# Multiplying by the values one group earlier in banded attention, and splitting the first projection weights on other engines and at other times

## The chip, the cores and the metric

The kernel runs as one program on one core of a Trainium2 chip. The metric is the device time of one execution in microseconds. The engines are PE (matrix products, with PEld for its weight loads), DVE (vector), ACT (scalar), POOL (GpSimd) and SP, which here only issues DMAs. Each engine takes its own instructions in order and meets the others through semaphores.

## The reference

Three layers follow one another. The first is what the change touches most: attention with a band of 96 keys and 8 global keys. The second mixes four attention experts, the third is an MLP.

```python
scores = scale * q @ k^T;  scores += -slope_h * distance
a = softmax(where(is_global | is_local, scores, -1e9))
x = a @ v                                  # B=2, H=8, S=768, D=64
for e in range(4):                         # second layer, D=512, Hd=64
    q, k, v = x @ wq[e], x @ wk[e], x @ wv[e]
    ye = softmax(causal(scale * q @ k^T)) @ v @ wo[e]
    out += gate_e * ye                     # top 2 of 4
u = out + mixed(out);  result = u + relu(u @ w_ch1) @ w_ch2
```

## The kernel before

**The work of the first layer.** Two heads make a pair and eight pairs are worked through. The 768 queries of a pair are six tiles of 128, each called a unit, so there are 48 units (`N_UNIT`); two units make a duo, and there are 24 duos (`N_DUO`). The band of a unit is 256 keys wide, except for the first unit of a pair, which has 128. So of every three duos the first is a little smaller.

**The stages of a duo.** PE computes scores (`scores`, line 1228). DVE adds the bias and takes the row minimum of the negated scores (`attend`, line 844). ACT takes the exponential and the sum (line 609). DVE inverts the sum (`safe` and `inverse`, lines 869 and 875) and POOL multiplies by the inverse (`divide`, line 545). PE transposes (`transposes`, line 1241) into `ps_t`. Each unit is then copied from `ps_t` to `probT`: this is `evac`, line 618 on ACT for every fourth unit and line 862 on DVE for the other three. So a duo of even number has one evacuation on each of the two engines, and a duo of odd number has both on DVE. PE multiplies by the values (`values`, line 1261) into `ps_o`, and ACT and DVE write the result to `xh` (line 630) and `xl` (line 882), its rounded part and the rest, since all later products take a sum of three products of such halves (`split_product`, line 1209).

**The order around the change.** It is written out by hand as one loop over `d` on each engine, and each engine runs through its own iterations `d`. Iteration `d` of PE holds `scores` of duo `d`, `values` of duo `d-4` and `transposes` of duo `d-2`, in that order. Iteration `d` of DVE holds the evacuations of duo `d-3`, the four `attend` of duo `d`, the inverse for duo `d-1`, and `x_lo` of duo `d-5`. Iteration `d` of ACT holds its evacuation for duo `d-3`, `x_hi` of duo `d-5` and the exponentials of duo `d`.

**The end of the layer.** From iteration 24 on PE interleaves the first projections of the second layer: keys from `wk` and then queries from `wq`, each for queries 0 to 511 (`LO`) and 512 to 767 (`HI`), by `project_first`. Then come eight transposes of `wo` (line 1484) and the value projections.

**The weights.** A weight comes by DMA to `wraw` or `nat`, and is split in a rounded and a remaining part: `split` on POOL, a cast (line 503) and a subtraction (line 495). The first halves of `wk` and `wq` are four such splits, put between POOL's divisions by `SPLIT_AT`. `wl_done` counts finished splits, so the constants `WK_0`, `WQ_0`, `WV` and so on name how many must be done. SP loads keys and values of pair `p` in turn and puts the weights between them.

Of the kernel before, what the change touches and what calls it, by code (L numbers as in the profile page):

```python
# [21 lines left out]
P = 128  # L22
# [110 lines left out]
def build(nc, t, out):  # L133
    ctx = ExitStack()
    with ctx:
# [145 lines left out]

        def by_unit(x):

            return x.rearrange("p k (f n) -> p k f n", f=2)
# [25 lines left out]
        woT_done, woT_hi, woT_lo = sem("woT_done"), sem("woT_hi"), sem("woT_lo")  # L310
        w1_in = [sem("w1_in0"), sem("w1_in1")]
# [30 lines left out]
        def _(sp):  # L342
# [43 lines left out]
            def load_first_weights():  # L386

                load_qk("wk", qk_first, 0, 0, wk_in)
                load_qk("wq", qk_first, P, 0, wq_in)
                load_wv()  # L390

            def load_late_weights():

# [13 lines left out]
            sp.dma_start(ident[:, :], t["ident"]).then_inc(ident_in, 16)  # L407
            load_values(0)
            load_keys(1)
            load_values(1)  # L410
            with sp.If(is_narrow(sp)):
                for p in range(2, B * HP):
                    load_keys(p)
                    load_values(p)
                    if p == 3:
                        load_first_weights()
                    elif p == 5:
                        load_constants()
                load_late_weights()
            with sp.Else():  # L420
                load_first_weights()
# [33 lines left out]
            def load_w1(j):  # L455

                if j == 0:
                    sp.wait_ge(wl_done, WQ_0)
# [34 lines left out]
        def _(pool):  # L493
# [3 lines left out]
            rqk = wraw[:, 0, 0:KT * 256].rearrange("p (k n) -> p k n", k=KT)  # L497
# [9 lines left out]
            def split_weight(n):  # L507

                if n < WQ_0:

                    of_q = n // 2
                    pool.wait_ge(wq_in if of_q else wk_in, 16)
                    k = slice(2 * (n % 2), 2 * (n % 2) + 2)
                    split(n, rqk[:, k, of_q * P:(of_q + 1) * P], qk_h[:, k, 1 - of_q, 0:P], qk_l[:, k, 1 - of_q, 0:P])
                elif n < WV:
                    k = n - WQ_0
# [32 lines left out]
            pool.wait_ge(one_done, 1)  # L549
            with pool.If(is_narrow(pool)):  # L550
                for d in range(N_DUO + 1):
                    if 1 <= d <= N_DUO:
                        divide(d - 1)
                    if d in SPLIT_AT:
                        split_weight(SPLIT_AT[d])
                pool.wait_ge(norm_done, 2 * N_UNIT)
            with pool.Else():
                for n in range(WQ_0):
                    split_weight(n)
            for n in range(WQ_0, WQK_1):  # L560
# [44 lines left out]
        def _(act):  # L605
# [1059 lines left out]
```

## Time and profile before

| | us |
|---|---|
| median of the runs | 455.48 |
| lowest and highest of three | 455.08, 455.73 |
| the profiled execution, own time | 455.48 |
| its span | 453.7 |
| PE busy | 441.6 (97%) |
| DVE, ACT, POOL busy | 188.5, 166.4, 174.8 |
| chain that ended last, on PE | 95% |

The profiled execution took as long as the median. Its span leaves out 1.8 us around the work. The duos of the first layer run up to about 76 us from the span's start, the interleaved projections to 91, the experts to about 210 and the MLP to the end. Busy time of PE is modelled from pipelined records, so 100% busy in a stretch does not by itself say that PE could go no faster; the start times of its groups say more.

### The profile page before, as it was taken

Reading aid. Unit: us, or ns where it says so; the run is one execution under the profiler, and the core shown is the slowest. Engines: PE = TensorE matmul, PEld = TensorE weight load, DVE = VectorE, ACT = ScalarE, POOL = GpSimd, SP = SyncE. Lnnn points to the kernel's source line nnn. Section 1 sums busy time; section 2 is a strip of 40 time slices with the busy share of each in tenths; the row PEclk is TensorE's granted clock in tenths of the full one; section 3 lists DMA queues with packets and bytes.
Section 4 is the critical chain, followed back from the end, with each engine's and each line's share of the span. In section 5 each row is a group of like instructions: output and inputs, shape, how many; then the busy total and the mean of one; then the engine's idle time right before and its main releaser. Section 6 shows DMA issues by size and latency. Waiting matters only on the chain.

```text
span 453.7 us, 8487 instructions
## 1 busy us (share of the span) xinstructions
PE 441.6 (97%) x3194; PEld 367.8 (81%) x3194; DVE 188.5 (42%) x615; ACT 166.4 (37%) x451; POOL 174.8 (39%) x247
## 2 busy tenths in 40 slices
PE   4999999999999999999999999999999999999996
PEld 3677777887787887667998888888888888888885
DVE  5799998265533634553351222221222122222112
ACT  4898886142643644756331011111012101111102
POOL 0777788806951555775011212222211121122210
PEclk9999999999999999999999999999999999999999
DMA  8797981100020011110101011110111022311003
GB/s 264 231 278 241 265 247 48 49 2 0 4 93 0 1 48 48 46 48 1 48 23 48 25 46 46 48 44 29 46 46 48 2 92 92 94 47 48 25 0 139
DMA packets 29949, 33.47 MB, mean 74 GB/s; under 512 B 9204, under 2 KB 19444, under 8 KB 29908
## 3 DMA queue, kind: packets, MB, share of 16 engines
q1 hardware_dynamic: 29474, 32.40, 23.9%
q8 instruction: 26, 0.43, 0.4%
q10 hardware_dynamic: 434, 0.52, 0.3%
q14 instruction: 15, 0.12, 0.1%
HBM read 29.77 MB, written 3.15 MB: 73 GB/s over the span
## 4 chain that ended last, share of the span: by engine, by line
PE 95%; ACT 1%; DMA 1%; issue 1%; DVE 1%; SPq 0%; POOL 0%; ACTq 0%
PE ps_s L1209 27%; PE ps_o L1209 25%; PE ps_t L1209 12%; PE ps_t L1241 5%; PE ps_s L1228 5%; PE ps_o L1261 5%; PE ps_s L1440 5%; PE ps_o L1473 4%; PE ps_t L1456 4%; PE ps_o L1385 1%; DMA kT<-in_k 1%; DVE prob L844 0%; ACT probT L681 0%; PE ps_o L1374 0%; ACT prob L609 0%
## 5 line engine op out<-in xcount | busy, mean ns | idle before, releaser
L495 POOL TENSOR_TENSOR fl<-fraw,fh 128x512 fp32r<-128x512 f32 x32 | 41.3, 1292 | 177.9 <-DVE fh L1151 177.9
L793 ACT ACTIVATE hidh<-ps_o 128x768 fp32r<-128x768 f32 x32 | 26.0, 813 | 175.8 <-PE ps_o L1209 175.8
L609 ACT ACTIVATE prob<-prob,smin 128x256 f32<-128x256 f32 (+3 forms) x144 | 77.6, 541 | 33.5 <-DVE smin L844 32.8
L1192 DVE SCALAR_TENSOR_TENSOR hidl<-ps_o,hidh 128x768 fp32r<-128x768 f32 x32 | 30.6, 957 | 93.0 <-ACT hidh L793 93.0
L545 POOL TENSOR_SCALAR prob<-prob,sinv,one 128x256 f32<-128x256 f32 (+1 forms) x96 | 50.5, 540 | 24.3 <-DVE sinv L875 24.1
L572 POOL TENSOR_SCALAR prob<-prob,sinv,gate 128x128 f32<-128x128 f32 (+5 forms) x48 | 34.0, 717 | 53.0 <-DVE sinv L895 52.9
L1209 PE MATMUL ps_s<-hidh,fl 128*128 128x512 f32 x128 | 50.4, 394 | 0.0
L1209 PE MATMUL ps_s<-hidl,fh 128*128 128x512 f32 x128 | 50.2, 392 | 0.0
L1209 PE MATMUL ps_s<-hidh,fh 128*128 128x512 f32 x128 | 49.7, 388 | 0.0
L1151 DVE CAST fh<-fraw 128x512 fp32r<-128x512 f32 x32 | 14.4, 449 | 66.5 <-PE ps_t L1209 66.4
L1209 PE MATMUL ps_o<-xh,w_late 128*128 128x512 f32 (+1 forms) x160 | 41.6, 334 | 0.0
L844 DVE CUSTOM_DVE_ANT_0 prob<-ps_s,bias 128x256 f32<-128x256 f32 (+1 forms) x96 | 34.4, 397 | 6.2 <-PE ps_s L1228 5.9
L844 DVE CUSTOM_DVE_ANT_0 prob<-ps_s,causal 128x128 f32<-128x128 f32 (+5 forms) x48 | 29.2, 614 | 18.7 <-PE ps_s L1440 11.9
L1209 PE MATMUL ps_t<-hidh,fh 128*128 128x256 f32 x128 | 35.3, 276 | 0.0
L1209 PE MATMUL ps_t<-hidl,fh 128*128 128x256 f32 x128 | 35.3, 276 | 0.0
L1209 PE MATMUL ps_t<-hidh,fl 128*128 128x256 f32 x128 | 35.3, 276 | 0.0
L681 ACT ACTIVATE probT<-ps_t 128x512 f32<-128x512 f32 (+1 forms) x48 | 24.2, 539 | 21.1 <-PE ps_t L1456 21.1
L1228 PE MATMUL ps_s<-kT,qT 64*128 64x256 f32 (+1 forms) x192 | 28.5, 423 | 2.9 <-DMA kT<-in_k 2.9
L1209 PEld LDWEIGHTS ps_o<-xh,w_late 128*128 128x128 f32 x160 | 28.6, 188 | 3.2
L1209 PEld LDWEIGHTS ps_t<-hidl,fh 128*128 128x128 f32 x128 | 24.0, 188 | 5.4
L1209 PEld LDWEIGHTS ps_t<-hidh,fh 128*128 128x128 f32 x128 | 24.0, 188 | 5.2
L1209 PEld LDWEIGHTS ps_s<-hidh,fl 128*128 128x128 f32 x128 | 24.1, 188 | 4.8
(180 smaller groups left out, 976.8 us busy)
## 6 DMA issues: line engine op xcount, KB each, us to landing
fraw<-in_w SPq DMA_DIRECT2D x32, 256.0 KB, 2.6
wraw<-in_w SPq DMA_DIRECT2D x8, 512.0 KB, 3.3
kT<-in_k SPq DMA_DIRECT2D x16, 224.0 KB, 3.8
vN<-in_v SPq DMA_DIRECT2D x8, 384.0 KB, 4.1
out<-prob SPq DMA_DIRECT2D x12, 256.0 KB, 2.7
qT<-in_q SPq DMA_DIRECT2D x7, 384.0 KB, 3.3
vB<-in_v SPq DMA_DIRECT2D x8, 192.0 KB, 4.2
kT<-in_k SPq DMA_DIRECT2D x7, 128.0 KB, 3.4
```

Source lines behind the costliest of these rows:

```text
L495: return pool.tensor_tensor(lo, raw, hi.bitcast(F32), ALU.subtract)
L545: pool.tensor_scalar(x, x, sinv[:, s:s + 1], one[:, 0:1], ALU.mult, ALU.mult).then_inc(norm_done, 1)
L572: pool.tensor_scalar(x, x, sinv[:, col + par:col + par + 1], gate[:, NT * b + i, e:e + 1], ALU.mult, ALU.mult).then_inc(mnorm_done, 1)
L609: act.activation(prob_s, prob_s, ACT.Exp, bias=smin[:, col:col + 1], scale=-1.0, accum_out=ssum[:, col:col + 1]).then_inc(done, 1)
L681: act.activation(flat[:, n0 * P:n1 * P], ps_t[:, g % 2, 0:(n1 - n0) * P], ACT.Copy).then_inc(mevac_done, 1)
L793: act.activation(hidh[:, f % 2, :], ps_o[:, 0:S], ACT.Relu).then_inc(hidh_done, 1)
L844: dve.tensor_tensor_reduce(out=dst, in0=src, in1=mask, scale=-SCALE, scalar=3e38, op0=ALU.add, op1=ALU.min, accum_out=smin[:, col:col + 1] ...
L1192: dve.scalar_tensor_tensor(hidl[:, f % 2, :], ps_o[:, 0:S], 0.0, hidh[:, f % 2, :].bitcast(F32), ALU.max, ALU.subtract).then_inc(hidl_done, 1)
L1209: last = pe.matmul(dst, a, m, start=start and k == 0, stop=stop and k == n - 1, **kw)
L1228: pe.matmul(a_score[s % 8][:, 0:keys.stop - keys.start], qT[half, p % 2, i * P:(i + 1) * P], kT[half, p % 2, keys], start=True, stop=True, ...
L1241: last = pe.transpose(ps_t[:, u % 2, (n * par + j) * P:(n * par + j + 1) * P], a_prob[s % 12][:, j * P:(j + 1) * P], ident[:, :])
L1261: last = pe.matmul(ps_o[half, at:at + P], v, a_probT[u % 4][:, par, n * P:(n + 1) * P], start=n == 0, stop=own, skip_group_check=True)
```

## The change

Four things change together.

1. `values` of a duo moves one iteration earlier on PE, to `d-3`; `x_hi` and `x_lo` follow, to `d-4`, and the loops on PE, DVE and ACT are one iteration shorter. The evacuations stay where they were, in iteration `d` for duo `d-3`.
2. The two projections `(0, HI)` and `(1, LO)` now stand side by side in iteration 25.
3. The two splits of `wk` are made by POOL before its first division, and the DMA of `wk` is issued before the values of pair 0. The split of `wq` leaves POOL: ACT makes the rounded part in one instruction and DVE the rest in one, both in iteration 24.
4. The constants are loaded after pair 3 and all late weights after pair 4; the cast `mix_hi` on DVE comes one iteration later.

```diff
-WO_BEHIND = {0: (12, 13), 1: (14, 15), VMIX_BEHIND: (16,)}
-WK_0, WQ_0, WV, WQK_1, WO, VMIX = 2, 4, 8, 12, 16, 17
-SPLIT_AT = {13: 0, 16: 1, 19: 2, 22: 3}
+WO_BEHIND = {0: (10, 11), 1: (12, 13), VMIX_BEHIND: (14,)}
+WK_0, WV, WQK_1, WO, VMIX = 2, 6, 10, 14, 15
...
             load_keys(0)
             sp.dma_start(ident[:, :], t["ident"]).then_inc(ident_in, 16)
+            load_qk("wk", qk_first, 0, 0, wk_in)
             load_values(0)
...
                     if p == 3:
-                        load_first_weights()
-                    elif p == 5:
                         load_constants()
-                load_late_weights()
+                    elif p == 4:
+                        load_late_weights()
...
                 if j == 0:
-                    sp.wait_ge(wl_done, WQ_0)
+                    sp.wait_ge(wl_done, WK_0)
+                    sp.wait_ge(wq_lo, 1)
...
             pool.wait_ge(one_done, 1)
+            for n in range(WK_0):
+                split_weight(n)
             with pool.If(is_narrow(pool)):
                 for d in range(N_DUO + 1):
                     if 1 <= d <= N_DUO:
                         divide(d - 1)
-                    if d in SPLIT_AT:
-                        split_weight(SPLIT_AT[d])
...
+            def split_wq_hi():
+                act.wait_ge(wq_in, 16)
+                act.activation(wqk_h[:, :, 0:P], wq_raw, ACT.Copy).then_inc(wq_hi, 1)
...
-                for d in range(N_DUO + 5):
+                for d in range(N_DUO + 4):
                     if 3 <= d < N_DUO + 3 and by_act(2 * (d - 3)):
                         evac(2 * (d - 3))
-                    if d >= 5:
-                        x_hi(d - 5)
+                    if d >= 4:
+                        x_hi(d - 4)
+                    if d == N_DUO:
+                        split_wq_hi()
...
+            def split_wq_lo():
+                dve.wait_ge(wq_hi, 1)
+                dve.tensor_tensor(wqk_l[:, :, 0:P], wq_raw, wqk_h[:, :, 0:P].bitcast(F32), ALU.subtract).then_inc(wq_lo, 1)
...
-                    if d >= 5:
-                        x_lo(d - 5)
+                    if d >= 4:
+                        x_lo(d - 4)
                     if d == N_DUO:
+                        split_wq_lo()
+                    elif d == N_DUO + 1:
                         mix_hi()
...
-                    pe.wait_ge(wl_done, WQ_0 if of_q else WK_0)
+                    pe.wait_ge(*((wq_lo, 1) if of_q else (wl_done, WK_0)))
...
-            first = {N_DUO: [(0, LO)], N_DUO + 1: [(0, HI)], N_DUO + 2: [(1, LO)], N_DUO + 3: [(1, HI)]}
+            first = {N_DUO: [(0, LO)], N_DUO + 1: [(0, HI), (1, LO)], N_DUO + 2: [(1, HI)]}
...
-                for d in range(N_DUO + 4):
+                for d in range(N_DUO + 3):
...
-                    if d >= 4:
-                        values(d - 4)
+                    if d >= 3:
+                        values(d - 3)
```

The order on PE from iteration 3 on, before: `ps_s<-kT,qT` are scores, `ps_t<-ident,prob` transposes and `ps_o<-probT` the product with the values.

```order
L1228 MATMUL ps_s<-kT,qT 128x128 x2
L1228 MATMUL ps_s<-kT,qT 128x256 x2
L1241 MATMUL ps_t<-ident,prob 128x128 x8
L1228 MATMUL ps_s<-kT,qT 128x256 x4
L1261 MATMUL ps_o<-probT,vN 64x128 x6
L1241 MATMUL ps_t<-ident,prob 128x128 x8
```

And the same place with the change, where line numbers are 11 higher:

```order
L1239 MATMUL ps_s<-kT,qT 128x128 x2
L1239 MATMUL ps_s<-kT,qT 128x256 x2
L1272 MATMUL ps_o<-probT,vN 64x128 x6
L1252 MATMUL ps_t<-ident,prob 128x128 x8
L1239 MATMUL ps_s<-kT,qT 128x256 x4
L1272 MATMUL ps_o<-probT,vB 64x128 x2
```

The values of duo 0 moved ahead of the transposes of duo 1, and so for each later duo: between the transposes of a duo and its product with the values there is now one group of scores, where before a whole iteration of three groups lay between them as well.

On DVE, iterations 24 to the end of the loop, before:

```order
L869 TENSOR_SCALAR seps<-ssum 128x4
L875 RECIPROCAL sinv<-seps 128x4
L882 TENSOR_TENSOR xl<-ps_o,xh 128x256
L900 CAST vmix<-vraw 96x768
L862 COPY probT<-ps_t 128x512
L882 TENSOR_TENSOR xl<-ps_o,xh 128x256
L862 COPY probT<-ps_t 128x512 x2
L882 TENSOR_TENSOR xl<-ps_o,xh 128x256 x3
```

and with the change:

```order
L872 TENSOR_SCALAR seps<-ssum 128x4
L878 RECIPROCAL sinv<-seps 128x4
L885 TENSOR_TENSOR xl<-ps_o,xh 128x256
L908 TENSOR_TENSOR wqk_l<-wraw,wqk_h 128x4x128
L865 COPY probT<-ps_t 128x512
L885 TENSOR_TENSOR xl<-ps_o,xh 128x256
L903 CAST vmix<-vraw 96x768
L865 COPY probT<-ps_t 128x512 x2
L885 TENSOR_TENSOR xl<-ps_o,xh 128x256 x2
```

The remaining part of `wq` came in ahead of an evacuation, the cast of `vmix` moved behind it, and one `xl` of the tail moved into the loop.

On POOL, from its memsets to the first divisions, with the change:

```order
L544 MEMSET one 128x1
L500 CAST wqk_h<-wraw 128x2x128
L492 ISA
L492 TENSOR_TENSOR wqk_l<-wraw,wqk_h 128x2x128
L500 CAST wqk_h<-wraw 128x2x128
L492 TENSOR_TENSOR wqk_l<-wraw,wqk_h 128x2x128
L337 TENSOR_LOAD narrow
L337 ISA x2
L548 COMPARE_AND_BRANCH
L541 ISA
L541 TENSOR_SCALAR prob<-prob,sinv,one 128x128 x2
```

Before, the load of `narrow` and the branch followed the memset at once; now two casts and two subtractions, which wait for the DMA of `wk`, stand ahead of them and of the first division.

## Rows read from the trace of the kernel before

**Rows 1.** Busy time by stretch: start:end, length, PE, PEld, DVE, ACT, POOL, PEclk, DMA, GB/s.

```profile
40.76:75.51 34.75, 34.75 (x361) 26.53 (x362) 32.48 (x151) 29.51 (x115) 29.08 (x56) 1.00 0.73 205
```

**Rows 2.** Timeline of PE, products with the values: start, duration, instructions.

```profile
47.55 0.44 PE L1261 MATMUL ps_o<-probT,vB 128*64 128x128 f32 x4
...
50.23 0.44 PE L1261 MATMUL ps_o<-probT,vB 128*64 128x128 f32 x4
...
53.34 0.88 PE L1261 MATMUL ps_o<-probT,vN 128*64 128x128 f32 x12
...
56.24 0.44 PE L1261 MATMUL ps_o<-probT,vB 128*64 128x128 f32 x4
...
58.92 0.44 PE L1261 MATMUL ps_o<-probT,vB 128*64 128x128 f32 x4
...
62.03 0.88 PE L1261 MATMUL ps_o<-probT,vN 128*64 128x128 f32 x12
```

**Rows 3.** Timeline of DVE: evacuations, and first attends, with idle time before them.

```profile
46.61 1.28 DVE L862 COPY probT<-ps_t 128x512 f32<-128x512 f32 x2
...
49.65 0.68 DVE L862 COPY probT<-ps_t 128x512 f32<-128x512 f32 x1
...
51.95 1.29 DVE L862 COPY probT<-ps_t 128x512 f32<-128x512 f32 x2
53.44 0.42 DVE L844 CUSTOM_DVE_ANT_0 prob<-ps_s,bias 128x256 f32<-128x256 f32 x1 [0.21 <-PE ps_s L1228]
...
58.19 1.01 DVE L862 COPY probT<-ps_t 128x256 f32<-128x256 f32 x2
...
61.08 0.69 DVE L862 COPY probT<-ps_t 128x512 f32<-128x512 f32 x1 [0.28 <-PE ps_t L1241]
```

**Rows 4.** Timeline of ACT: its evacuations in the same stretch.

```profile
50.24 0.36 ACT L618 ACTIVATE probT<-ps_t 128x256 f32<-128x256 f32 x1
...
55.89 0.57 ACT L618 ACTIVATE probT<-ps_t 128x512 f32<-128x512 f32 x1
```

**Rows 5.** Timelines of PE in two iterations: the transposes of a full duo.

```profile
19.26 1.23 PE L1241 MATMUL ps_t<-ident,prob 128*128 128x128 f32 x8
...
25.19 1.09 PE L1241 MATMUL ps_t<-ident,prob 128*128 128x128 f32 x8
```

**Rows 6.** The chain that ended last: start, duration, what; the two `HI` projections.

```profile
80.33 1.42 PE ps_s L1209 x12
...
87.35 1.61 PE ps_s L1209 x12
```

**Rows 7.** The start: SP's issue of ident, and ident's time to landing.

```profile
3.56 0.51 SPq L407 DMA_DIRECT2D ident<-in_ident  x1
...
DMA to landing us min/median/max: 4.5/4.5/4.5
```

**Rows 8.** The start: SP's last issue of keys of pair 1, and its time to landing.

```profile
7.66 0.47 SPq L360 DMA_DIRECT2D kT<-in_k  x1
...
DMA to landing us min/median/max: 5.4/5.5/5.6
```

**Rows 9.** Busy time by stretch, columns as in rows 1, at the start.

```profile
8.00:12.00 4.00, 3.71 (x16) 2.47 (x16) 2.12 (x13) 3.14 (x14) 0.23 (x1) 1.00 1.08 333
```

**Rows 10.** The start: timelines of DVE, POOL and PE, with idle time before.

```profile
4.74 0.42 DVE L907 TENSOR_SCALAR near<-rel,cnt 128x384 f32<-128x384 f32 x1 [1.07 <-DMA kpos<-in_kpos]
...
11.77 4.11 POOL L545 TENSOR_SCALAR prob<-prob,sinv,one 128x128 f32<-128x128 f32 x8 [10.79 <-DVE sinv L875]
...
14.39 1.65 PE L1228 MATMUL ps_s<-kT,qT 64*128 64x128 f32 x8
```

**Rows 11.** Timeline of POOL: one weight split, a cast and a subtraction.

```profile
74.44 0.40 POOL L503 CAST wqk_h<-wraw 128x256 fp32r<-128x256 f32 x1
74.92 0.74 POOL L495 TENSOR_TENSOR wqk_l<-wraw,wqk_h 128x256 fp32r<-128x256 f32 x1
```

**Rows 12.** Timeline of DVE in iteration 25: the evacuation, with idle time before it.

```profile
80.36 0.69 DVE L862 COPY probT<-ps_t 128x512 f32<-128x512 f32 x1 [2.62 <-PE ps_t L1241]
```

More of the change, by code:

```diff
@@ L280, in mixed_part @@
             return lambda x: x[:, :, HI], ps_fill.rearrange("p (c n) -> p c n", c=EP)
+        wq_raw = wraw[:, 0, 0:KT * 256].rearrange("p (k n) -> p k n", k=KT)[:, :, P:2 * P]
         def by_unit(x):
@@ L310, in build @@
         woT_done, woT_hi, woT_lo = sem("woT_done"), sem("woT_hi"), sem("woT_lo")
+        wq_hi, wq_lo = sem("wq_hi"), sem("wq_lo")
         w1_in = [sem("w1_in0"), sem("w1_in1")]
@@ L384, in load_wv, with load_late_weights @@
                 sp.dma_start(dst[:, :, 256:260], t["w_gate"]).then_inc(wv_in, 16)
-            def load_first_weights():
-                load_qk("wk", qk_first, 0, 0, wk_in)
+            def load_late_weights():
                 load_qk("wq", qk_first, P, 0, wq_in)
                 load_wv()
-            def load_late_weights():
                 load_qk("wk", qk_raw, 0, 1, wqk_in)
@@ L495, in lo_of @@
                 return pool.tensor_tensor(lo, raw, hi.bitcast(F32), ALU.subtract)
-            rqk = wraw[:, 0, 0:KT * 256].rearrange("p (k n) -> p k n", k=KT)
+            rk = wraw[:, 0, 0:KT * 256].rearrange("p (k n) -> p k n", k=KT)
             rv = wraw[:, 1, 0:KT * 260].rearrange("p (k n) -> p k n", k=KT)
@@ L507, in split_weight @@
             def split_weight(n):
[L509 to L514, printed above, removed]
+                if n < WK_0:
+                    pool.wait_ge(wk_in, 16)
+                    k = slice(2 * n, 2 * n + 2)
+                    split(n, rk[:, k, 0:P], qk_h[:, k, 1, 0:P], qk_l[:, k, 1, 0:P])
                 elif n < WV:
-                    k = n - WQ_0
+                    k = n - WK_0
                     pool.wait_ge(wv_in, 32)
@@ L553, in _ @@
                         divide(d - 1)
-                    if d in SPLIT_AT:
-                        split_weight(SPLIT_AT[d])
                 pool.wait_ge(norm_done, 2 * N_UNIT)
             with pool.Else():
-                for n in range(WQ_0):
-                    split_weight(n)
-            for n in range(WQ_0, WQK_1):
+                pool.drain()
+            for n in range(WK_0, WQK_1):
                 split_weight(n)
@@ L659, in _ @@
                 act.drain().then_inc(evac_act, ACT_EVACS)
+                split_wq_hi()
             def take_queries():
@@ L924, in _ @@
                 head_bias(0)
-                for d in range(N_DUO + 5):
+                for d in range(N_DUO + 4):
                     if 3 <= d < N_DUO + 3:
@@ L992, in _ @@
                 dve.drain().then_inc(evac_dve, N_UNIT - ACT_EVACS)
+                split_wq_lo()
             def take_keys():
```

1 line of the change is left out of this document (removed).

## The prediction

> **What bounds the kernel now.** I read the stretches first, then the chain of waits, then the timelines of the four engines over two rounds of the attention loop. PE is busy in all of 34.75 us of the loop, DVE in 32.48, ACT in 29.51 and POOL in 29.08 [rows 1]. Since busy time of PE is modelled, I checked it by starts. The value products of iterations 16 and 19 start at 53.34 and 62.03, 8.69 us apart, and so are those of 14 and 17 and of 15 and 18 [rows 2]. DVE waits for PE's scores in this stretch, 0.21 us in iteration 16 [rows 3]. So PE sets the pace of the loop and DVE follows closely, with 32.48 of 34.75 us (93%). After the loop PE runs on almost without a gap to the end. Each instruction that the change moves on PE is executed before and after, so only waits and switches of PE can change the time. What PE waits more in the loop is not made up for later.
>
> I number PE's iterations by the value products of rows 2: iteration 14 at 47.55, 15 at 50.23, 16 at 53.34, 17 at 56.24, 18 at 58.92, 19 at 62.03.
>
> **The change part by part.**
>
> *The value products, one iteration earlier.* Now they need the evacuations of iteration `d` itself, on DVE and ACT. Before, they used those of `d-1`, and the first to need the new ones were the transposes, about 1.0 us later. I compare each start in rows 2 with the end of the evacuations of the same iteration. I allow 0.04 us for the step from the end on another engine to PE's start, an estimate.
>
> - Iteration 14: DVE's pair ends at 46.61 + 1.28 = 47.89 [rows 3]. PE comes at 47.55: late by 0.38.
> - 15: ACT ends at 50.60 [rows 4], DVE at 50.33 [rows 3], PE comes at 50.23: late by 0.41.
> - 16: DVE ends at 51.95 + 1.29 = 53.24, PE comes at 53.34: not late.
> - 17: ACT ends at 55.89 + 0.57 = 56.46, PE comes at 56.24: late by 0.26.
> - 18: DVE ends at 58.19 + 1.01 = 59.20, PE comes at 58.92: late by 0.32.
> - 19: DVE ends at 61.77, PE comes at 62.03: not late.
>
> These must not simply be added, as a wait on PE moves the later scores, but what DVE and ACT do from earlier scores does not move. I carry it. Iteration 14 pays 0.38. In 15 the evacuations hang on the scores of 14, issued before that wait, so they stay, while PE comes 0.38 later: it pays 0.41 - 0.38 = 0.03. In 16 and 17 everything is 0.41 later, since DVE waits for PE's scores there [rows 3]; 16 pays nothing, and 17 pays 0.26. In 18 the evacuations hang on scores that moved by 0.41, PE has moved by 0.67: it pays 0.32 - 0.26 = 0.06. In 19 nothing. The sum is 0.73 us in six iterations. Such waits can arise in iterations 5 to 23, 19 of them, or 3.2 times six: **2.3 us lost**. What is queued behind a waiting product is the next transposes and scores, and for these POOL's output and DVE wait. The bounds: 1.37 x 3.2 = 4.4 us if each lateness is paid in full, and 0.41 if PE, once late, stays behind the evacuations for good.
>
> *The fill of the loop.* Before, the transposes of duo 1 and 2 partly wait for POOL: those at 19.26 take 1.23 us, later ones of the same shape 1.09 [rows 5]. With a value product ahead of them this wait is filled: 0.14 gained, between 0 and 0.5.
>
> *The `HI` and `LO` projections side by side.* A `HI` after a value product took 1.61 us, one after transposes 1.42 [rows 6]. The change has one such switch less: 0.19 gained, between 0 and 0.3.
>
> *POOL's four splits out of the loop.* Each is 0.40 + 0.74 us with a gap of 0.08 [rows 11]. POOL is busy for 29.08 of 34.75 us [rows 1] and PE never waits for it in the loop, so taking them out is worth nothing.
>
> *`wk` at the start.* Its DMA goes out right after `ident`, which was issued at 3.56 and landed at 8.06 [rows 7]. 256 KB at 333 GB/s [rows 9] are 0.8 us, so `wk` lands at about 8.9. Two splits take 2 x 1.22 - 0.08 = 2.4 us to 11.3, and then POOL must still load `narrow` and branch. No row shows that by itself. DVE did it in its 1.07 us of idle time before 4.74 [rows 10], so it is between 0 and 1.07, and POOL is ready between 11.3 and 12.4. Its first division started at 11.77 [rows 10], on the chain. So the loss is between 0 and 0.6; I take 0.1, nearer the low end, as DVE's idle time was ended by a DMA and is a wide bound. The loads behind `wk` come 0.8 us later: the keys of pair 1 landed at 7.66 + 5.5 = 13.2 [rows 8] and are then there at 14.0, ahead of PE's 14.39 [rows 10]. So that costs nothing, and 0.3 us if the short rows of `wk` go at half the rate.
>
> *`wq` on ACT and DVE.* One copy of 512 columns on ACT (0.57, the evacuation of that width in [rows 4]) and a subtraction on DVE, at most the 2 x 0.74 of POOL's two [rows 11]. DVE has 2.62 us of idle time before the next evacuation there [rows 12], from 77.74 on, and PE needs the queries' weights only after the first `HI`, at 80.33 + 1.42 = 81.75 [rows 6]. Nothing; without that cover it would be about 1 us. The first load of `w1` waits some 3 us longer for its buffer, and POOL splits `w1` only from 117 us on: nothing. The same for the constants and late weights, which SP issues earlier than before they are needed.
>
> **Sum:** 2.3 - 0.14 - 0.19 + 0.1 = 2.1 us. The profiled execution took 455.48 us (span 453.7, 1.8 around it), which is also the median: **457.6 us**.
>
> **A rule of the skill against the trace.** In [rows 1] PE is busy 34.75 of 34.75 us, its weight loads 26.53, or 76%. The Trainium skill (Perfetto Trace Analysis, section Identifying the Most-Contended Engine) calls matmul busy time a bad measure and the share of weight loads a good one. By it PE would have room in the loop, and the shorter pipeline could use it; that is the fifth rival. The equal spacing of PE's starts speaks for PE being at its limit all the same.
>
> **The rivals.**
>
> 1. *PE pays once.* If PE, once 0.41 us late, stays behind the evacuations, the time is 455.48 + 0.41 - 0.33 + 0.1 = 455.7, no change. For it: a wait in one iteration lowers the lateness in the next. Against it: DVE and ACT start each iteration from PE's scores, so they are pushed along. It decides from the point where DVE no longer waits for the scores (its idle time of 0.21 in iteration 16 gone). Chance 0.14.
> 2. *Every lateness is paid.* Then 4.4 - 0.33 + 0.1 = 4.2 us: 459.7. For it: DVE, at 93%, has little to catch up with, and 0.05 us on each of its steps adds more than half a microsecond. Chance 0.11.
> 3. *The start slips.* POOL reaches its first division 0.6 us late and the keys of pair 1 are late by 0.3: 458.5 with my forecast for the rest. Chance 0.08.
> 4. *The clock falls in the loop.* The granted clock is 1.00 there [rows 1], its upper level of 2.4 GHz, with PE never idle. With about 0.1 us of wait in each iteration it could fall to the lower one, and a round of three duos would take up to 17.4 us and not 8.69 [rows 2]: one such round makes 466. Chance 0.02. The Trainium skill (TensorE: Matmul & The Clock Gate, section A second HAM failure mode: psum-queue depth-cycling) tells of short idle times between groups of matmuls that lower the clock; no row here shows it.
> 5. *Faster, and the one on the other side.* If the round of 8.69 us is set by a loop of dependencies through DVE and `ps_o` rather than by PE's own work, taking one iteration out of the way of the values lets it shrink to DVE's share: 2.27 us of 34.75 [rows 1], or 3.7 us over the 57 us of the loop: 451.8. It decides from PE having any hidden gap. Against it speak the constant spacing and DVE's waits for PE. Chance 0.07, fills of the start that are larger than I think included.
>
> **How the numbers follow.** The forecast has the remaining 0.58, with its own range of 456.3 to 458.9. A measurement of this kernel can tell about 0.2%, or 0.9 us, from no change. Slower by more than that are most of the forecast (0.55), rivals 2 to 4 (0.21): 0.76. Within it are rival 1 and the low end of the forecast: 0.17. Faster is rival 5: 0.07. The range reaches from rival 1 to rival 2, 455.6 to 459.7; outside are rivals 4 and 5 and tails.
>
> **What would show it.** Right: in PE's timeline idle time before value products, of 0.2 to 0.4 us in some iterations, released by `probT` on DVE for pairs and on ACT otherwise; about 2.3 us in all between 15 and 76 us; rounds of three duos 0.3 to 0.4 us longer than 8.69; POOL's first division still near 11.8; no wait for `wq`. Wrong: rounds that stay at 8.69 (rival 1), grow by 0.7 (rival 2) or shrink (rival 5), or a first division past 12.2 (rival 3). The projections and everything behind 91 us should only be shifted; if time is gained or lost there, I have missed a dependency.

## The result, and the profile after

| | median of the runs | range | profiled execution | its span |
|---|---|---|---|---|
| before | 455.28 us | 454.75 to 455.73 | 455.48 us | 453.7 us |
| changed | 458.77 us | 458.44 to 459.3 | 458.41 us | 456.6 us |

The changed kernel is slower: ratio 1.0066, 95% interval 1.0046 to 1.0087. The ratio is over more executions than the table: the 18 of the changed kernel have a mean of 458.30 us, 3.0 us over before, where the medians of four differ by 3.5. The forecast was 457.6 us, in a range of 455.6 to 459.7. The direction, and where the time is lost, came out as predicted; the loss is 2.9 us between the profiled executions, where 2.1 were forecast.

The page of the profile after has one line that answers at once: the chain that ended last. Before, 95% of it were PE's. After:

```profile
PE 89%; DVE 4%; issue 3%; ACT 2%; DMA 1%; SPq 0%; POOL 0%; DVEq 0%; ACTq 0%
```

Between 20 and 80 us the chain now passes through evacuations, DVE's in most iterations and ACT's in some early ones. Next, the stretches. Two rounds of three duos in the middle of the loop, the kernel before:

```profile
43.60:60.97 17.37, 17.37 (x182) 13.18 (x181) 16.16 (x75) 14.74 (x58) 14.81 (x29) 1.00 0.94 254
...
120.00:220.00 100.00, 98.55 (x847) 77.51 (x847) 42.89 (x152) 54.68 (x135) 56.56 (x70) 1.00 0.11 35
```

and the same two stretches of the changed kernel (columns as in [rows 1]; the first is what it needs for the same 182 matmuls):

```profile
43.30:61.50 18.20, 17.63 (x182) 13.25 (x182) 16.60 (x77) 14.83 (x59) 12.50 (x25) 1.00 0.79 239
...
120.00:220.00 100.00, 98.55 (x837) 76.71 (x838) 44.63 (x156) 55.33 (x137) 58.98 (x73) 1.00 0.10 33
```

Two rounds took 17.37 us, all of it busy. They take 18.20 now, of which 17.63 are busy. Behind the loop PE is busy for 98.55 of 100 us in both. The last transposes before the second layer's value projections, by which I mark the end of the attention part, stand at

```profile
89.91 1.09 PE L1484 MATMUL ps_t<-ident,o 128*128 128x128 f32 x8
```

before, and in the changed kernel at

```profile
92.80 1.09 PE L1495 MATMUL ps_t<-ident,o 128*128 128x128 f32 x8
```

That is 2.89 us later, and the span is 2.9 us longer. All of the loss lies ahead of this mark.

Where in the loop? These rows of PE's timeline answer [rows 2], in iterations 14, 16 and 18 of the changed kernel: scores, then the value products, which wait.

```profile
49.27 1.14 PE L1239 MATMUL ps_s<-kT,qT 64*128 64x256 f32 x8
50.56 0.44 PE L1272 MATMUL ps_o<-probT,vB 128*64 128x128 f32 x4 [0.15 <-DVE probT L865]
...
55.13 1.14 PE L1239 MATMUL ps_s<-kT,qT 64*128 64x256 f32 x8
56.37 0.44 PE L1272 MATMUL ps_o<-probT,vB 128*64 128x128 f32 x4
...
61.32 0.93 PE L1239 MATMUL ps_s<-kT,qT 64*128 64x128 f32 x8
62.56 0.88 PE L1272 MATMUL ps_o<-probT,vN 128*64 128x128 f32 x12 [0.31 <-DVE probT L865]
```

The number in brackets is the idle time that the modelled ends leave, and it is too small. By starts: full scores take 1.06 us to the next group where nobody waits, those of the smaller duos 0.85. Here they take 1.29, 1.24 and 1.24. So PE waits 0.23, 0.18 and 0.39 us, in iterations 14, 16 and 18. DVE's evacuations, which answer [rows 3]:

```profile
49.18 1.28 DVE L865 COPY probT<-ps_t 128x512 f32<-128x512 f32 x2
...
55.00 1.27 DVE L865 COPY probT<-ps_t 128x512 f32<-128x512 f32 x2
...
61.44 1.01 DVE L865 COPY probT<-ps_t 128x256 f32<-128x256 f32 x2
```

They end at 50.46, 56.27 and 62.45, and PE's products start at 50.56, 56.37 and 62.56: 0.10 to 0.11 us behind them each time. Where ACT's evacuation ends last, PE starts 0.05 to 0.06 us behind it. Counted so over all iterations, PE waits 0.86 us in every six from iteration 12 on, 1.41 in iterations 4 to 11, and 3.14 in all.

### The profile page after: what moved, and what is told of

Same layout as the page of the kernel before. It is cut to its first block, busy times and chain, and to the rows that moved or that the text cites. A ratio compares the mean times of both kernels' runs of the same rounds, so it can differ in the third digit from the quotient of the medians.

```text
span 456.6 us, 8488 instructions
## 1 busy us (share of the span) xinstructions
PE 442.3 (97%) x3194; PEld 368.0 (81%) x3194; DVE 190.8 (42%) x616; ACT 167.1 (37%) x452; POOL 173.1 (38%) x243
## 4 chain that ended last, share of the span: by engine, by line
PE 89%; DVE 4%; issue 3%; ACT 2%; DMA 1%; SPq 0%; POOL 0%; DVEq 0%; ACTq 0%
PE ps_s L1220 27%; PE ps_o L1220 25%; PE ps_t L1220 12%; PE ps_s L1451 5%; PE ps_o L1484 4%; PE ps_t L1467 4%; PE ps_o L1272 3%; PE ps_s L1239 3%; PE ps_t L1252 3%; DVE probT L865 1%; PE ps_o L1396 1%; ACT prob L604 1%; DMA kT<-in_k 1%; DVE prob L847 1%; DVE smin L847 0%
## 5 line engine op out<-in xcount | busy, mean ns | idle before, releaser
L1162 DVE CAST fh<-fraw 128x512 fp32r<-128x512 f32 x32 | 14.4, 450 | 66.8 <-PE ps_t L1220 66.8
```

## The experiments

Each trace is cut at two marks that don't depend on modelled ends: the start of the scores of iteration 6, and the transposes of `o` at the end of the attention part. Where the values come a duo early, one product (1.03 us) has moved ahead of the first mark, so it is taken off the first column. From mark to mark the kernel before takes 66.60 us. With the values early and no wait it would be 66.60 - 1.03 - 0.19 (one switch less, [rows 6]) = 65.38 us. "Lost" is what a kernel with early values (changed, e2 to e5, e9 to e11) is over 65.38, and one with late values over 66.60. For most kernels this is time that PE waits; in e8 a lower clock adds to it. Behind the second mark all fourteen kernels take the same, 363.7 to 363.9 us.

| kernel | first mark | mark to mark | lost | ratio to before | 95% interval |
|---|---|---|---|---|---|
| before | 23.31 | 66.60 | 0 | 1 | |
| changed | 23.77 | 68.00 | 2.62 | 1.0066 | 1.0046 to 1.0087 |
| e1 values late | 23.96 | 67.75 | 1.15 | 1.0053 | 1.0026 to 1.0080 |
| e2 values only | 23.91 | 68.94 | 3.56 | 1.0086 | 1.0065 to 1.0107 |
| e3 wait per unit, swap | 24.39 | 66.54 | 1.16 | 1.0042 | 1.0019 to 1.0066 |
| e4 wait per unit | 24.85 | 67.45 | 2.07 | 1.0064 | 1.0040 to 1.0087 |
| e5 biases on POOL | 24.16 | 70.72 | 5.34 | 1.0137 | 1.0109 to 1.0165 |
| e6 `wk` early only | 24.45 | 66.61 | 0.01 | 1.0022 | 1.0007 to 1.0037 |
| e7 values late, old loads | 24.26 | 66.60 | 0 | 1.0010 | 0.9994 to 1.0027 |
| e8 load order only | 23.44 | 70.75 | 4.15 | 1.0076 | 1.0048 to 1.0105 |
| e9 swap, old loads | 24.37 | 66.54 | 1.16 | 1.0012 | 0.9996 to 1.0029 |
| e10 changed, old loads | 25.64 | 68.02 | 2.64 | 1.0060 | 1.0038 to 1.0082 |
| e11 no late biases | 24.19 | 67.89 | 2.51 | 1.0050 | 1.0032 to 1.0069 |
| e12 block behind keys | 24.52 | 67.24 | 0.64 | 1.0017 | 0.9996 to 1.0037 |

Marks and "lost" are of one execution each. The ratios are of several, each against the runs of before beside it. Most intervals are some 0.2% wide to each side, or 0.9 us, so smaller differences between kernels rest on the marks alone.

**Theory and rivals.** The theory: all that is lost are waits of the value products for evacuations of their own iteration. Rivals: it is another part of the change (loads, `wk` at the start, the splits), or the values cost something that no wait shows.

**e1: the values put back.** The changed kernel with value products, products of `x` and projections in the places of before; all else stays.

```diff
-                    if d >= 3:
-                        values(d - 3)
+                    if d >= 4:
+                        values(d - 4)
```

> The changed kernel with one part undone: the product with the values is back at duo d-4, with x_hi and x_lo at d-5 and the first projections one by one. All moves of weights, splits and loads stay. My theory (the 3.5 us come from PE waiting for the evacuations of the same iteration): 455.3 us, the time of before within 0.3 us, the value products in the loop again 8.69 us apart for three duos, no idle time of PE between 19 and 76 us. Rival (the early load of wk, POOL's splits at the start, or wq on ACT and DVE cost a part): 456.5 us or more, with the first division on POOL or the projections late.

The waits before value products are gone, and rounds are of 8.69 us again. But the time has not come back: ratio 1.0053. One row of PE holds nearly all of the 1.15 us lost between the marks:

```profile
51.15 0.93 PE L1239 MATMUL ps_s<-kT,qT 64*128 64x128 f32 x8 [1.05 <-DMA kT<-in_k]
```

These are the first scores of pair 5, and they wait for keys. So another part of the change has a price of its own, which the changed kernel's trace doesn't show. The first mark is 0.65 us later as well, and the twelve runs scatter from 456.41 to 462.23 us. It is taken up in e7, e8 and e10.

**e2: only the values early,** with the two products side by side, made in the kernel before. `wk` and `wq` are loaded and split as before, POOL's four splits stand in the loop.

```diff
-                    if d >= 4:
-                        values(d - 4)
+                    if d >= 3:
+                        values(d - 3)
```

> The kernel before with one part of the change alone: values at duo d-3, x_hi and x_lo at d-4, (0, HI) and (1, LO) side by side. The four splits stay between POOL's divisions and the loads where they were. My theory: the whole loss, 458.2 to 458.8 us, with six duos taking 18.2 us in place of 17.4. Rival (POOL's splits taken out of the loop had paid for a part, so that without this it is worse): above 459.5. Rival (the loss comes from the weights): within 0.5 us of before.

Its ratio is 1.0086 against 1.0066 for the changed kernel, with intervals that overlap. The marks tell them apart: it loses 3.56 us between them instead of 2.62. The waits of the changed kernel are all there, and in iterations 15, 18 and 21, behind three of the splits, they are 0.40, 0.88 and 0.39 us where that had 0.06, 0.39 and 0.07. Timelines of POOL, DVE and PE at iteration 18:

```profile
60.89 0.73 POOL L495 TENSOR_TENSOR wqk_l<-wraw,wqk_h 128x256 fp32r<-128x256 f32 x1
...
60.92 0.72 DVE L869 TENSOR_SCALAR seps<-ssum 128x4 f32<-128x4 f32 x1
...
62.30 1.01 DVE L862 COPY probT<-ps_t 128x256 f32<-128x256 f32 x2
...
63.41 0.88 PE L1261 MATMUL ps_o<-probT,vN 128*64 128x128 f32 x12 [0.81 <-DVE probT L862]
```

DVE's operation on four columns takes 0.16 to 0.17 us in most iterations (the median of 18 is 166 ns). Here it takes 0.72: it ends with POOL's subtraction, 0.55 us late, and the evacuation and PE are late in turn. At 51.62, 70.55 and 79.86, beside the other three splits, it is 0.72 to 0.73 again. The Trainium skill (SBUF — State Buffer, section Who interferes with whom) says that VectorE in some modes and GpSimd take a port by turns, for a whole instruction, and that the other is fully blocked. The trace agrees, with 0.72 beside 0.73.

**e4 and e3: other waits.** e4: the changed kernel, where each unit's products wait for that unit's evacuation alone. e3: e4, and ACT takes the second unit of the even duos instead of the first.

```diff
-                pe.wait_ge(*evac_of(2 * d))
-                pe.wait_ge(*evac_of(2 * d + 1))
...
+                    pe.wait_ge(*evac_of(u))
```

```diff
-    return u % 4 == 0
+    return u % 4 == 1
```

> The same without the exchange on ACT: each unit's value product waits for its own evacuation, ACT keeps the first unit of even duos. My theory: the waits of odd duos (both evacuations on DVE) go, those of even duos, where ACT's evacuation of the first unit is the late one, stay: 0.8 us faster than the changed kernel, 458.0 us. Rival: as for the one before, 458.3 to 458.8.

> The changed kernel, where the value product of each unit waits only for the evacuation of that unit (before: both units of the duo ahead of the first product), and where ACT evacuates the second unit of a duo of even number in place of the first. Nothing is left out. My theory (what counts is how many tenths of a us an evacuation is late, 0.1 to 0.4 each time, and the second unit's product starts 0.5 us after the first): most waits go, 2.0 us faster than the changed kernel, 456.5 to 457.0 us. Rival (DVE at 93 per cent sets a slower pace of its own once the pipeline is shorter): no more than 0.5 us faster, 458.3.

Between the marks e4 loses 2.07 us and e3 1.16, where the changed kernel loses 2.62. That is 0.55 and 1.46 less, where 0.8 and 2.0 were expected. In e4 the waits of odd duos are gone as expected, but PE then comes sooner and those of even duos grow, to 0.33 us in iteration 15 and 0.16 in 17, where they were 0.06 and 0.01. What remains in e3 is for the most part hidden inside the value products. In its twin e9 a group of twelve takes 1.16 us instead of 0.88, as its second unit waits for ACT:

```profile
34.89 0.58 ACT L618 ACTIVATE probT<-ps_t 128x512 f32<-128x512 f32 x1
35.02 1.16 PE L1276 MATMUL ps_o<-probT,vN 128*64 128x128 f32 x12
```

By starts, the value products of e9 between the marks are about 1.1 us longer than those of before, which is nearly all of its 1.16. In e3 they are about 0.95 longer, and its transposes at 51.15 take 1.02 us to the next group instead of 0.80: scores of pair 5 wait 0.22 us for keys, as in e1. So the waits are the loss, and nothing is left for a cost of early values that no wait shows. The ratios move less than the marks, 1.0064 and 1.0042. Both traces have a later first mark, 24.85 and 24.39, which fits, but isn't shown for the runs without a trace.

**e5: the head biases of ScalarE given to GpSimd.** In the iterations 5 and 7 the changed kernel waits 0.44 and 0.41 us. Its rows of ACT and PE there, a bias in front of the evacuation that PE waits for:

```profile
21.93 0.51 ACT L619 ACTIVATE bias<-dist 128x384 f32<-128x384 f32 x1
22.35 0.57 ACT L613 ACTIVATE probT<-ps_t 128x512 f32<-128x512 f32 x1
```

```profile
22.98 0.44 PE L1272 MATMUL ps_o<-probT,vB 128*64 128x128 f32 x4 [0.36 <-ACT probT L613]
```

```diff
-                    if d < X_PARTS * (HP - 1) and d % X_PARTS in (0, 1):
+                    if d < 2:
                         head_bias(2 * (d // X_PARTS) + 2 + d % X_PARTS)
```

and on POOL, behind the divisions of `d` = 4, 5, 7 and 8, the four biases.

> The changed kernel, with the four head biases that ScalarE makes for heads 4 to 7 made by GpSimd instead. If the waits of 0.44, 0.41 and 0.28 us that TensorE has in the iterations 5, 7 and 9 (slots 21.5, 27.5, 33.9 us) come from a head bias of 0.42 to 0.51 us that stands ahead of ScalarE's evacuation, a term my sum left out, they shrink to about 0.1 each: 0.4 us less in all than in the changed kernel, ratio about 1.0057 where that had 1.0066, and the rest of its waits (0.86 in every six iterations) stay. If the lateness of ScalarE comes from the evacuation itself, nothing moves. The edit's own risk: GpSimd's divisions come one bias later, and then the transposes wait instead.

A miss, by the edit and not by the question: POOL runs behind, and DVE waited 3.5 us for two of the biases.

```profile
27.84 0.29 DVE L851 CUSTOM_DVE_ANT_0 prob<-ps_s,bias 128x128 f32<-128x128 f32 x1 [1.53 <-POOL bias L554]
```

It says little of ACT's part: only iteration 5 lies ahead of that wait, and there PE's wait falls from 0.44 to 0.02 us.

**e11: these four biases left out.**

> The changed kernel without the four head biases that ScalarE makes inside the loop (heads 4 to 7 take those of heads 0 to 3 in the first layer, so this part of the result is left out). The run with these biases on GpSimd didn't answer, since VectorE waited 3.5 us for them. If a bias ahead of ScalarE's evacuation makes the waits of 0.44 and 0.41 us in the iterations 5 and 7, they are 0.05 to 0.2 here, and the kernel takes 0.4 to 0.7 us less than the changed kernel: ratio 1.005 to 1.006, first value projections of layer 2 at 93.2 to 93.5 us where it has 93.9. If the biases have no part, the waits stay at 0.4.

The wait of iteration 5 falls from 0.44 to 0.07 us and that of 7 from 0.41 to nothing. The biases made them. But 6, 8 and 10 now have 0.33, 0.22 and 0.22 where they had 0.05, 0 and 0.18: PE comes sooner and meets DVE's evacuations. Over the iterations 4 to 11 that is 0.91 us instead of 1.41, so half a microsecond is the biases' part. The ratio, 1.0050 against 1.0066, agrees with that but couldn't show it alone. The first value projections stand at 94.2 us and not at 93.2 to 93.5, since the start of this execution was slower.

**e7, e8, e10: the loads.** e8 is the kernel before with one edit, in the order in which SP issues:

```diff
                     if p == 3:
-                        load_first_weights()
-                    elif p == 5:
                         load_constants()
-                load_late_weights()
+                    elif p == 4:
+                        load_first_weights()
+                        load_late_weights()
```

> The kernel before, with one edit: the constants are loaded behind pair 3, and all late weights (2.3 MB) in one block behind pair 4, ahead of the keys of pair 5. In the run with the values late, TensorE waited 1.05 us for keys that were issued behind that block. If the block causes it, the same wait of about 1 us stands here before the scores of one duo between 47 and 52 us, and the kernel takes 0.7 to 1.2 us longer, ratio 1.002. In the changed kernel the same keys were needed 1.2 us later, and nobody waited. If it was chance of that run, no wait, ratio 1.000.

The mechanism was right, and the size four times what I expected. SP's timeline: the first weight of the block, `wo` at its end, and behind it the keys of pair 5.

```profile
36.73 0.56 SPq L376 DMA_DIRECT2D wraw<-in_wk  x1
...
41.96 0.87 SPq L396 DMA_DIRECT2D o<-in_wo  x1
42.87 0.62 SPq L355 DMA_DIRECT2D qT<-in_q  x1
43.54 0.43 SPq L356 DMA_DIRECT2D kT<-in_k  x1
```

PE's rows in iteration 15, and its granted clock behind the wait:

```profile
48.71 0.87 PE L1241 MATMUL ps_t<-ident,prob 128*128 128x128 f32 x6
52.08 1.65 PE L1228 MATMUL ps_s<-kT,qT 64*128 64x128 f32 x8 [2.50 <-DMA kT<-in_k]
53.66 0.69 PE L1261 MATMUL ps_o<-probT,vB 128*64 128x128 f32 x4
```

```profile
53.00:54.00 1.00, 1.00 (x8) 0.35 (x8) 0.24 (x3) 0.00 (x0) 0.00 (x0) 0.50 1.11 330
```

The transposes take 3.37 us to the next group instead of 0.80: 2.57 are the wait. Behind it the granted clock is 0.50, its lower level of 1.2 GHz, and the scores and value products take 1.58 and 1.87 instead of 0.85 and 1.03: 1.57 more. Together 4.14 of the 4.15 us. That is one execution; the twelve runs scatter from 456.94 to 462.98 us, so the wait isn't the same each time.

e7 is e1 with the loads in the order of before, but for `wk`:

```diff
                     if p == 3:
-                        load_constants()
-                    elif p == 4:
                         load_late_weights()
+                    elif p == 5:
+                        load_constants()
+                load_last_weights()
```

> The run with the values late again (value products, products of x and projections in the order of before), and the weights and constants loaded in the order of before, but for wk, which stays at the start. What is left of the change is the early wk, wq split by ScalarE and VectorE, and no splits of GpSimd in the loop. If the block of weights and the start made the 0.5% of that run, this one has the start alone: 0.1 to 0.9 us over before, ratio 1.000 to 1.002, and the difference to the run with wk early alone is nought. If ScalarE's and VectorE's split of wq costs, this one is over that run by 0.5 us or more, with a wait of TensorE between 72 and 80 us.

Its loop, as one stretch:

```profile
25.00:75.00 50.00, 50.00 (x520) 38.00 (x520) 46.85 (x214) 43.34 (x167) 36.47 (x71) 1.00 0.79 221
```

It loses nothing between the marks, and its ratio of 1.0010 can't be told from 1. So `wq` on ACT and DVE costs nothing that can be seen, and the 0.5% of e1 were, in the main, the load order.

e10 is the changed kernel with the edit of e7:

> The changed kernel with the weights and constants loaded in the order of before (wk stays at the start). In the kernel before, the new order alone cost 0.76% (a wait of 2.50 us for the keys of pair 5 and the slow clock behind it), with the old order and the values late 0.1% were left. In the profile of the changed kernel nobody waits for those keys: the waits for evacuations, 1.6 us by then, have put off the need for them. If the two costs hide each other so, this kernel takes what the changed kernel takes, ratio 1.006 to 1.007, and its trace shows the same waits before the value products, 3.1 us in all. Rival, that the profiled run was a lucky one and the block of weights costs in most others: ratio 1.003 to 1.005, clearly under the changed kernel.

Ratio 1.0060 and 2.64 us lost: what the changed kernel has. In the profiled execution of that kernel the load order costs nothing, since its scores of pair 5 are due so late:

```profile
52.39 0.93 PE L1239 MATMUL ps_s<-kT,qT 64*128 64x128 f32 x8
```

In e8 the keys were there by 52.04, and it wanted them at 49.5. In the changed kernel they landed at 51.43, 0.96 us before they were wanted. The waits for evacuations, and the product that has moved ahead, cover the wait for keys. The rival, a lucky profiled run, finds no support in the ratios, but intervals of 0.2% to each side leave room for a part of it.

**e9: e3 with the loads of before** is the best form of the change that I know.

> The run with one wait per unit and ScalarE taking the second unit of the even duos, with the old order of loads (wk stays at the start). Its loop had next to no waits with the values early. If the order of loads made the rest of its 0.42%, this one comes to the start's price less what the change was to bring (HI and LO side by side 0.19, fill 0.14): ratio 0.9995 to 1.0015, and it would be the best form of the change, level with before. If it stays at 1.003 or more, the values a duo earlier cost something that neither the waits nor the loads show.

Ratio 1.0012, interval 0.9996 to 1.0029. It takes back most of the loss, and no gain is shown: it still waits 1.16 us between the marks, and the side-by-side products and the filled start bring back 0.33 at most. No version here is shown to be faster than the kernel before. Between e3 and e9 the marks are alike, and the intervals of their ratios overlap, so what the old load order is worth in this form stays open.

**e6: only `wk` at the start,** in the kernel before, with its two splits ahead of POOL's first division.

```diff
             sp.dma_start(ident[:, :], t["ident"]).then_inc(ident_in, 16)
+            load_qk("wk", qk_first, 0, 0, wk_in)
```

> The kernel before, with one edit: wk is loaded behind the identity at the start, and its two splits stand ahead of GpSimd's divisions. The first batch had the first transposes at 12.62 to 13.30 us where before has 12.36 and the changed kernel 12.46. If the early weights cause that (256 KB ahead of the keys of pair 1), they start here at 12.5 to 13.3 too, and the kernel takes 0.1 to 0.9 us longer, ratio 1.000 to 1.002; the granted clock may show 0.5 for some microseconds behind the first transposes, as in three runs of the first batch, and this would cost little, since TensorE waits for GpSimd there. Rival, that the start only scatters from run to run: ratio within 0.9995 to 1.0005, and the first transposes within 12.3 to 12.6.

Ratio 1.0022, and nothing lost between the marks. But the first transposes stand at 12.33, where the kernel before has 12.36, so neither the expectation nor its rival fits as a whole. What is late is the first mark, 24.45 instead of 23.31. PE's weight loads show why. Scores of iteration 4 in the kernel before, and then in e6:

```profile
17.38 0.73 PEld L1228 LDWEIGHTS ps_s<-kT,qT 64*128 64x128 f32 x8 [0.17 <-issue]
```

```profile
17.85 1.36 PEld L1230 LDWEIGHTS ps_s<-kT,qT 64*128 64x128 f32 x8 [0.33 <-DVE smin L846]
```

Eight loads take 0.73 us in one and 1.36 in the other. In every trace PE works at about half its rate for some microseconds between the first transposes and the first mark. In the kernel before that is over by 17.4 us, in e6 it lasts until after 19 us. How long it lasts differs from run to run, with `wk` early or not.

**e12: the block behind the keys of pair 5,** again in the kernel before, with `wk` in the block.

```diff
                     if p == 3:
-                        load_first_weights()
+                        load_constants()
                     elif p == 5:
-                        load_constants()
-                load_late_weights()
+                        load_first_weights()
+                        load_late_weights()
```

> The kernel before with the constants behind pair 3, as in the run with the load order alone, but the block of late weights (2.3 MB) behind the keys and values of pair 5 instead of ahead of them; wk comes in the block. If the wait of 2.50 us for keys in that run came from standing behind the block, there is none here: the keys of pair 5 are issued near 39 us as in the kernel before, those of pair 6 behind the block, near 50 us, 9 us or more before their scores. Ratio 0.999 to 1.001, loop without waits, and the first transposes at 12.3 to 12.7 us, since wk isn't at the start. If the block itself takes the DMA engines from all that lands between 45 and 55 us, a wait of 0.5 us or more for keys of pair 6 or values of pair 5 stands at 50 to 62 us, ratio 1.002 or more.

The wait of 2.50 us is gone, and 0.64 us are lost in its place, at the keys of the next pair:

```profile
59.91 0.93 PE L1228 MATMUL ps_s<-kT,qT 64*128 64x128 f32 x8 [0.56 <-DMA kT<-in_k]
```

```profile
49.20 2.67 SPq L396 DMA_DIRECT2D o<-in_wo  x1
51.91 0.69 SPq L355 DMA_DIRECT2D qT<-in_q  x1
```

SP took 2.67 us to issue `wo` at the end of the block, and came to the queries and keys of pair 6 at 51.91 us, where the kernel before does so at 49.55. So both halves of the expectation hold in part: the place of the block decides the large wait, the block itself a small one. This run also has the first transposes at 13.48 us, later than any other, without `wk` at the start. With e2 and e8 (12.62, 12.40) and before (12.36) the kernels without it range over 12.36 to 13.48, the ten with it over 12.33 to 13.30. Three of the four without it are at 12.62 or before, eight of the ten with it at 12.92 or behind. So a part of the delay may belong to `wk`; one execution each doesn't decide it.

The ten traces with `wk` at the start do show one price. Rows of POOL and DVE in the changed kernel, ahead of POOL's first division:

```profile
10.58 0.73 POOL L492 TENSOR_TENSOR wqk_l<-wraw,wqk_h 128x256 fp32r<-128x256 f32 x1
11.09 0.24 DVE L872 TENSOR_SCALAR seps<-ssum 128x4 f32<-128x4 f32 x1
```

The operation on four columns ends with POOL's subtraction again, as in e2. In all ten traces it ends 0.02 to 0.03 us behind the second subtraction, and it takes 0.24 to 0.60 us; in the four without `wk` there it takes 0.16 to 0.17. The first division needs its result, and so comes 0.08 us later in the changed kernel's profiled execution and up to 0.44 later in e9.

## Why the prediction was right, and where it was off

- **What bounds the kernel.** Right: PE. In the kernel before rounds are of 8.69 us with nothing idle, and in e7 too.
- **The values a duo earlier.** The kind of wait was right: waits for `probT` before value products, of up to 0.44 us, released by DVE for pairs and by ACT otherwise. I had 0.73 us in six iterations and 2.3 in all; the trace has 0.86 and 3.14. This is the term that was mis-sized, for two reasons. I allowed 0.04 us from the end of an evacuation to PE's start, which no row gave, and the rows show 0.10 to 0.11 behind DVE and 0.05 to 0.06 behind ACT; by hand, with 0.10 and 0.05, the sum of six becomes 0.82. And I spread six late iterations over the whole loop, where ACT has four head biases to make in the early ones. e11 puts those at 0.5 us.
- **The carrying by hand.** Right in that not each lateness is paid (rival 2 would be 4.4 us), but more than one (rival 1). Which iterations pay was wrong. I had 0.38 us in 14, 0.26 in 17 and 0.06 in 18; the trace has 0.23 in 14, 0.18 in 16, 0.01 in 17 and 0.39 in 18. I kept PE's arrival times of before. But with the change the small value product, which takes 0.81 us to the next group where a full one takes 1.03, stands in iterations 15 and 18, and no longer in 16 and 19:

```profile
53.30 0.88 PE L1272 MATMUL ps_o<-probT,vN 128*64 128x128 f32 x12
```

  From the scores of 15 to the values of 16 PE took 3.96 us before. Without its waits of 0.06 and 0.18 it takes 3.74 now, and so it meets an evacuation that had ended 0.10 us before PE came. That explains 16; with nothing paid in 17, the lateness of 18 is paid in full. That the sum came near all the same was partly luck. e11 shows the same once more, since a wait taken away in iteration 5 comes back in part in 6.
- **The fill, and the products side by side.** 0.14 and 0.19 were the gains forecast. Both are in the account of the profiled execution: 3.14 + 0.10 - 0.14 - 0.19 = 2.91, and 2.89 were measured at the mark.
- **POOL's splits out of the loop.** "Worth nothing" was wrong. POOL is not waited for, but its subtraction holds up DVE for 0.55 us, and DVE is waited for as soon as the values are early: e2 loses 0.94 us more than the changed kernel. It did no harm to the sum. In the kernel before, POOL's four subtractions each start 0.02 or 0.16 us after DVE's operation has begun, and the operation takes 0.16 to 0.17 us. So its evacuations end where they end in e7, which has no splits in the loop, to 0.02 us from iteration 6 on.
- **`wk` at the start.** 0.1 us in the profiled execution, as taken: first division at 11.86, before 11.77. But the reason was another. I asked when POOL would be ready; what came late was DVE's result, held up by POOL's subtraction, and in other traces it cost up to 0.44 us. What it costs on the average is open. e6 says 0.22% (0.07 to 0.37), e7 and e9, which also have it, 0.10% and 0.12% with 1 in their intervals, and e12 has 0.17% without it.
- **The constants and late weights "earlier than needed": nothing.** Right for the changed kernel's profiled execution, by luck. I looked at when they are needed themselves and not at what is queued behind them. e8 shows 4.15 us for that alone. In the changed kernel the cost is covered by the very waits that it brings.
- **`wq` on ACT and DVE.** Nothing, as e7 shows within 0.2%.
- **Rival 3**, the start slips: not in the profiled execution. Over all executions the kernels are 3.0 us apart and the profiled ones 2.9, so there is no rest to explain. Still, the first mark scatters from 23.31 to 25.64 us over the traces here, with a start that differs from execution to execution. Its 458.5 should read 458.4 by its own terms. **Rival 4**: the granted clock stayed at 1.00 in the loop, through all waits of up to 0.44 us. **Rival 5** fell, and with it what I had drawn from the rule of the Trainium skill (Perfetto Trace Analysis, section Identifying the Most-Contended Engine): PE with 76% of weight loads had no room here.

## What to carry to other kernels

Before a consumer is moved a stage ahead in a pipeline, compare its start with the end of its producer in the same iteration, add the measured step between the engines (0.05 to 0.11 us here), check whether the groups ahead of the consumer are still as long as they were, and look through the producer's own queue for work that only some iterations have. Work on an engine that nobody waits for may still hold up one that is waited for, so check that engine's short instructions for outliers. A block of loads must be judged by what is queued behind it; and if two delays cover each other, undo each part alone, or the second is found only when the first has been mended.

## What the runs showed of the hardware

- From the end of an evacuation to the start of the matmul that waits for it: 0.10 to 0.11 us from DVE (50.46 to 50.56, 56.27 to 56.37, 62.45 to 62.56), 0.05 to 0.06 from ACT (22.92 to 22.98).
- A DVE operation on 4 columns went from 0.17 to 0.72 us, four times out of four in e2, beside a POOL subtraction of 0.73 that had begun 0.03 to 0.04 us before it. POOL's divisions, of one tensor each, do the same, for a shorter time: in the changed kernel the operation took 0.36, 0.37, 0.23, 0.37 and 0.23 us at 35.77, 44.91, 54.12, 63.13 and 72.34, and each time it ended 0.02 to 0.03 us behind a division. Not every overlap counts. Beside a subtraction that began 0.02 us after it (48.83 in the kernel before), and beside a division that had begun 0.08 us before it (33.82), it took 0.16 to 0.17.
- An idle time of PE of 2.5 us within a busy loop was followed by about 3.5 us at a granted clock of 0.50, which cost another 1.57. Waits of 0.44 us and less left it at 1.00 in the changed kernel, and so did one of 1.05 us in e1 and one of 1.66 in e5.
- The column of the granted clock seems to miss the lower level at the start. In eight of the fourteen traces it shows 0.50 for some microseconds between 14 and 20 us; in the other six, the kernel before and the changed one among them, it shows 1.00 there. But in the kernel before the weight loads of the scores at 14.4 us take 285 to 330 ns each and the matmuls 417 to 631, and at 17.4 us 182 to 187 and 376 to 480. In e8 behind its long wait, where the column says 0.50, the same loads take 282 to 330 and the matmuls 417 to 631. So durations have to be looked at as well.
- SP's issue of one load took 0.34 to 0.66 us in most cases (58 of 62 in the kernel before, between 12 and 75 us), and up to 2.67 in e12 and 2.78 in e11 in the block of late weights. The block of e8 and e12 is 2.1 MB by the sizes in the trace; the 2.3 of their expectations were too high.
